# A three-part fused kernel on one core: the bonus term of the recurrence as two dense products with ones from unit 6 on, and a few moved steps

## The chip, the cores and the metric

The kernel runs on one core of a Trainium2 chip. The metric is the device time of one execution in microseconds (us), as the median of several runs. The engines are called PE (matrix products), DVE (vector), ACT (scalar), POOL (GpSimd) and SP (which here issues nearly all DMAs). Each runs its own list of instructions in order and waits on semaphores.

## The reference

Three blocks follow each other, all in float32, with batch B = 2, 8 heads, S = 768 steps, head size D = 48 (8 x 48 = 384 = DM), DFF = 1024.

```
for t in range(S):                       # recurrence, per batch and head
    y[t]  = r[t] @ (state + outer(u * k[t], v[t]))
    state = w[t][:, None] * state + outer(k[t], v[t])
x = y of all heads, side by side         # (B, S, 384)

xk, xr = mu * x + (1 - mu) * x_prev      # two mixes with the step before
out1   = sigmoid(xr @ w_r) * (relu(xk @ w_k) ** 2 @ w_v)

h = gelu(out1 @ w_in);  u2, v2 = halves of h
v2 = layernorm(v2) * g;  v2 = w_sg @ v2 + b_sg      # mixes the 768 steps
result = out1 + (u2 * v2) @ w_out
```

The part of y[t] that comes from u is, per head, (sum over d of r[t,d] * u[d] * k[t,d]) times v[t]: one number per step and head, times a vector. This is what the kernel calls the bonus.

## The kernel before

**Units.** The recurrence is cut into 12 units: unit `un` is a chunk of C = 128 steps (`un // 2`) of one batch (`un % 2`). The 8 heads lie as 4 pairs; a pair fills the 128 partitions, each head in a slot of 64 (48 used, the rest zero). One operand of a unit is thus 128 x 512: 4 pairs side by side, 128 steps each. For each unit DVE runs two scans over the decays (`scan`: prod, suffix) and makes k_in and r_in from them; PE makes the scores (`scores`), the keys by step (`keys_by_step`, a transpose), the bonus (`bonus`), the part of the state (`from_state`), the new state (`add_state`) and the part of the chunk (`from_chunk`). `outputs` is bonus, from_state, add_state, from_chunk. DVE masks the scores (`mask`), multiplies the bonus by v (`bonus`), adds the outputs (`last_output`, `main_output`) and carries the state on (`carry_on`). The outputs of a pair's last part go through small DMAs into X.

**The bonus before.** POOL multiplies r by k (`products`, L577) into rkp. PE multiplies rkp from the left by a matrix that repeats u along its columns (`u_b`, part of the tile par), so that every row of the result holds the sum: 8 products a unit, one for each pair and head, 64 x 64 weights and 64 x 128 moving columns, in plain float32 (L694). The result goes to bank pkt, for units 0, 1 and 3 to other banks.

**Split numbers.** The large products of the second and third block are made of three products of float32r numbers each: a number is split in a high part (rounded by ACT) and a low part (number minus high, by POOL or DVE), and high x high, high x low, low x high are added. The groups named `_h` and `_l` are these. `low_part` and `low_half` make the low parts of weights, `key_low` those of the squared activations k2.

**Stages.** The first feed-forward block goes in 6 stages s of 256 columns (chunk s of both batches). A stage has tiles RS (2), KS (4), VS (2) in `first_mlp`. While stage s runs on PE, the units a = 2s+2 and b = 2s+3 are made, and mix(s+1) (ACT and DVE) prepares the inputs of the next stage out of X. So units 6 and 7 belong to stage 2, 10 and 11 to stage 4, and the bonus of unit 6 comes right after RS[0] of stage 2. Stage 5 has no unit. After it the third block follows (L323 to L325 on PE).

**Order.** Everything is in an order written out by hand for each engine: a loop over the stages with one branch for s = 0, s = 1, the middle stages and the last. Each helper begins with its waits. What waits is the whole engine: an ACT instruction that waits for POOL holds back what stands behind it on ACT.

## Time and profile before

| | us |
|---|---|
| median of 3 runs | 326.71 (326.59 to 328.05) |
| the profiled execution, device time | 327.06 |
| its span, first to last instruction | 325.3 |
| PE busy | 317.0 (97%), 2682 instructions |
| DVE busy | 197.6 (61%), 340 instructions |
| ACT busy | 151.4 (47%), 304 instructions |
| POOL busy | 94.2 (29%), 92 instructions |

A row of the timeline gives start, length, engine, line, what is written and read, and in square brackets the idle time in front of it with what ended it; rows of the same kind are merged ("x16"). Matmuls overlap: the length of one is from its first step to its last result (268 ns for one of L694), while the next starts 64 ns later. What a run of them costs is therefore read from start to start, or from the chain of waits, which gives each group only the time up to the next one. A float32 product appears as two records. The device time is 1.8 us above the span.

### The profile page before, as it was taken

How to read it: one execution, taken by the hardware profiler on the slowest of the kernel's cores; microseconds unless marked ns; L12 is line 12 of the kernel's file. 1: busy time of each engine (PE TensorE's matmuls, PEld its weight loads, DVE VectorE, ACT ScalarE, POOL GpSimd, SP SyncE). 2: the span in 40 equal slices, each digit the busy share in tenths (PEclk: the TensorE clock that was granted, in tenths of full speed). 3: DMA queues.
4: the chain of work that ended last, by engine and by line, in shares of the span. 5: the costliest groups of instructions: out<-in, count | busy, mean ns of one | idle time of the engine just before them, and what ended most of it. 6: DMA issues, size and time to landing. Idle time of an engine off the chain costs nothing.

```text
span 325.3 us, 6820 instructions
## 1 busy us (share of the span) xinstructions
PE 317.0 (97%) x2682; PEld 298.7 (92%) x2682; DVE 197.6 (61%) x340; ACT 151.4 (47%) x304; POOL 94.2 (29%) x92
## 2 busy tenths in 40 slices
PE   6989999999999999999999999999999999999996
PEld 2769889998999999999999998899999989999995
DVE  5979997979985498549217156982535456123332
ACT  6478805742554655385555884744113026311100
POOL 5430140263014301431131141671333019213220
PEclk9999999999999999999999999999999999999999
DMA  7996044004413403200024055000000300000012
GB/s 230 406 390 264 3 169 170 2 13 166 163 33 138 168 3 93 88 0 2 8 78 174 0 200 190 2 0 0 2 0 3 121 24 0 2 0 2 0 48 97
DMA packets 11172, 28.07 MB, mean 86 GB/s; under 512 B 1216, under 2 KB 6016, under 8 KB 9856
## 3 DMA queue, kind: packets, MB, share of 16 engines
q1 hardware_dynamic: 10848, 27.33, 23.7%
q8 instruction: 21, 0.34, 0.4%
q10 hardware_dynamic: 288, 0.27, 0.3%
q14 instruction: 15, 0.12, 0.1%
HBM read 24.74 MB, written 2.36 MB: 83 GB/s over the span
## 4 chain that ended last, share of the span: by engine, by line
PE 93%; DVE 3%; ACT 1%; issue 1%; POOL 1%; DVEq 0%; ACTq 0%; POOLq 0%
PE dense L780 35%; PE dense L325 5%; PE dense L323 5%; PE dense L324 5%; PE ps L665 4%; PE ps L323 3%; PE ps L325 3%; PE ps L324 3%; PE pkt L694 3%; PE py L734 3%; PE py L748 3%; PE dense L319 2%; PE pu L718 2%; PE pkt L323 2%; PE pkt L325 2%; PE pu L323 2%
## 5 line engine op out<-in xcount | busy, mean ns | idle before, releaser
L586 POOL TENSOR_TENSOR k_l<-sq,k_h 128x512 fp32r<-128x512 f32 x22 | 28.3, 1292 | 58.0 <-ACT sq L1045 58.0
L577 POOL TENSOR_TENSOR rkp<-inw 128x512 f32<-128x512 f32 x12 | 16.2, 1352 | 81.9 <-DVE r_in L1275 61.6
L780 PE MATMUL dense<-k_h,wv_h 128*128 128x256 f32 x144 | 39.1, 286 | 0.0
L780 PE MATMUL dense<-xkr_h,wk_h 128*128 128x256 f32 x144 | 38.7, 291 | 0.0
L780 PE MATMUL dense<-k_h,wv_l 128*128 128x256 f32 x144 | 38.7, 283 | 0.0
L780 PE MATMUL dense<-xkr_h,wk_l 128*128 128x256 f32 x144 | 36.1, 283 | 0.0
L780 PE MATMUL dense<-k_l,wv_h 128*128 128x256 f32 x144 | 32.9, 283 | 0.0
L780 PE MATMUL dense<-xkr_l,wk_h 128*128 128x256 f32 x144 | 30.4, 283 | 0.0
L645 POOL TENSOR_TENSOR gated_l<-gf,gated_h 128x384 fp32r<-128x384 f32 x16 | 16.4, 1025 | 46.1 <-ACT gated_h L1174 36.2
L1174 ACT CAST gated_h<-gf 128x384 fp32r<-128x384 f32 x16 | 8.2, 513 | 42.9 <-DVE gf L1523 42.9
L780 PEld LDWEIGHTS dense<-xkr_h,wk_h 128*128 128x128 f32 x144 | 27.5, 191 | 0.6 <-issue 0.2
L780 PEld LDWEIGHTS dense<-k_h,wv_h 128*128 128x128 f32 x144 | 27.6, 192 | 0.3 <-issue 0.2
L780 PEld LDWEIGHTS dense<-k_h,wv_l 128*128 128x128 f32 x144 | 27.6, 192 | 0.0
L780 PEld LDWEIGHTS dense<-xkr_h,wk_l 128*128 128x128 f32 x144 | 26.7, 192 | 0.0
L1336 DVE SCALAR_TENSOR_TENSOR xf<-X,omu,xf 128x256 f32<-128x256 f32 x36 | 18.8, 536 | 12.6 <-ACT xf L1003 12.6
L1037 ACT ACTIVATE relu<-dense 128x512 f32<-128x512 f32 x24 | 14.3, 595 | 25.3 <-PE dense L780 25.3
L780 PEld LDWEIGHTS dense<-k_l,wv_h 128*128 128x128 f32 x144 | 24.2, 192 | 0.0
L1003 ACT ACTIVATE xf<-X,par 128x256 f32<-128x256 f32 x36 | 17.6, 504 | 13.0 <-DMA X<-y 11.3
L780 PEld LDWEIGHTS dense<-xkr_l,wk_h 128*128 128x128 f32 x144 | 23.3, 192 | 0.0
L619 POOL TENSOR_TENSOR rstd<-vare,half_neg 128x1 f32<-128x1 f32 x12 | 9.3, 777 | 29.8 <-DVE vare L1501 29.8
L627 POOL TENSOR_TENSOR vn_l<-vf,vn_h 128x512 fp32r<-128x512 f32 x12 | 17.1, 1430 | 2.2 <-ACT vn_h L1135 2.2
L1013 ACT CAST xkr_h<-xf 128x256 fp32r<-128x256 f32 x36 | 14.3, 397 | 6.4 <-DVE xf L1336 6.4
(258 smaller groups left out, 876.0 us busy)
## 6 DMA issues: line engine op xcount, KB each, us to landing
inw<-in_units SPq DMA_DIRECT2D x10, 1026.5 KB, 5.4
vb<-in_vT SPq DMA_DIRECT2D x12, 256.0 KB, 5.9
wsg_raw<-in_wsgT SPq DMA_DIRECT2D x1, 2304.0 KB, 8.8
out_y<-y_out SPq DMA_DIRECT2D x12, 192.0 KB, 1.9
wk_raw<-in_moe_w_k SPq DMA_DIRECT2D x3, 512.0 KB, 9.7
wv_raw<-in_moe_w_v SPq DMA_DIRECT2D x4, 384.0 KB, 15.1
win_raw<-in_moe_w_in SPq DMA_DIRECT2D x3, 512.0 KB, 4.7
inw<-in_units SPq DMA_DIRECT2D x2, 512.0 KB, 5.2
```

The source lines that it names most:

```text
L323: pe.matmul(o, a_h, b_h, start=first and n == 0, stop=False, skip_group_check=True)
L324: pe.matmul(o, a_h, b_l, start=False, stop=False, skip_group_check=True)
L325: mm = pe.matmul(o, a_l, b_h, start=False, stop=last and n == len(pairs) - 1, skip_group_check=True)
L577: pool.tensor_tensor(rkp[:, un % 2], inw[:, un % 3, W1:W1 + WIDE], inw[:, un % 3, W1 + WIDE:W1 + 2 * WIDE], ALU.mult).then_inc(rkp_done, 1)
L586: pool.tensor_tensor(k2_l[:, 2 * n:2 * n + 2], sq[:, j % 2].rearrange("p (g t) -> p g t", g=2), k2_h[:, 2 * n:2 * n + 2], ALU.subtract).th ...
L627: pool.tensor_tensor(vn_l[:, t], vf[:, n % 2], vn_h[:, t], ALU.subtract).then_inc(vnl_done, 1)
L645: pool.tensor_tensor(gated_l[:, x, cols], gf[:, ng % 2], gated_h[:, x, cols], ALU.subtract).then_inc(gl_done, 1)
L780: return pe.matmul(pm[bk][:, n * T:(n + 1) * T], weight[:, t, cols], inputs[:, t], start=first, stop=last, skip_group_check=True)
L1003: act.activation(batches(xf[:, kt, n]), X[:, s % 2, kt, :, 1:C + 1], ACT.Identity, scale=mu[:, n, kt:kt + 1]).then_inc(t_done, 1)
L1013: act.copy(xkr_h[:, n, kt], xf[:, kt, n]).then_inc(xh_done, 1)
L1037: act.activation(relu[:, j % 2], pm[bk][:], ACT.Relu).then_inc(m_free[bk], 1)
L1336: dve.scalar_tensor_tensor(out=batches(xf[:, kt, n]), in0=X[:, s % 2, kt, :, 0:C], scalar=omu[:, n, kt:kt + 1], in1=batches(xf[:, kt, n]), ...
```

## The change

Four things are changed.

- From unit 6 on (WIDE_FROM = 3 * N = 6) POOL multiplies r by u (read with a repeated column) and then by k; ACT rounds the result to rk_h, POOL takes the rest rk_l = rkp - rk_h, written over rkp; PE then multiplies rk_h and rk_l, 128 x 512 each, by `heads`, a 128 x 128 matrix with ones where row and column belong to the same head and zeros elsewhere. These are two float32r products that add up in bank pkt. ACT writes heads once, in stage 0.
- PE: the bonus of unit 1 stands in front of move_last(0), and the keys of unit 3 in front of its bonus.
- DVE: the low parts of wv and the two carries carry_on(0), carry_on(1) stand later; one half of the low part of wk goes from DVE to POOL; one wait of unit 0's scan is placed an instruction later.
- Room: rk_h lies over `moves`, which is used in units 0 and 1 alone; p_sum, of a branch that does not run here, lies over z.

The diff, without some lines of the layout and the declarations:

```diff
--- before
+++ after
@@ SBUF layout
+        rk_at = e
         rkp, e = put("rkp", e, [2, WIDE])
+        rk_l, _ = put("rk_l", rk_at, [2, WIDE], FR)
...
-        moves, e = put("moves", e, [KT, P])
+        moves, _ = put("moves", e, [KT, P])
+        rk_h, e = put("rk_h", e, [2, WIDE], FR)
+        heads, e = put("heads", e, [P], FR)
...
@@ which engine splits which weight tile
-        POOL_LOWS = [("wr", 0, 0), ("wk", 0, 0)]
-        DVE_LOWS = [("wk", 1, 0), ("wk", 2, 0), ("wk", 0, 1), ("wk", 1, 1), ("wk", 2, 1)]
+        POOL_LOWS = [("wr", 0, 0), ("wk", 0, 0), ("wk", 0, 1)]
+        DVE_LOWS = [("wk", 1, 0), ("wk", 2, 0), ("wk", 1, 1), ("wk", 2, 1)]
@@ POOL
+            def weighted(un):
+
+                n = un - WIDE_FROM
+                pool.wait_ge(s_par, 16)
+                pool.wait_ge(rin_done, un + 1)
+                pool.wait_ge(c_mm, un - 1)
+                pool.tensor_tensor(blocks(rkp[:, un % 2]), blocks(inw[:, un % 3, W1:W1 + WIDE]),
+                                   u_b[:, :, 0:1].to_broadcast([P, PAIRS, C]), ALU.mult).then_inc(rku_done, 1)
+                pool.wait_ge(rku_done, n + 1)
+                pool.tensor_tensor(rkp[:, un % 2], rkp[:, un % 2],
+                                   inw[:, un % 3, W1 + WIDE:W1 + 2 * WIDE], ALU.mult).then_inc(rkp_done, 1)
+
+            def weighted_low(un):
+                pool.wait_ge(rkh_done, un - WIDE_FROM + 1)
+                pool.tensor_tensor(rk_l[:, un % 2], rkp[:, un % 2], rk_h[:, un % 2], ALU.subtract).then_inc(rkl_done, 1)
...
-            low_half(pool, parts_of("wk")[0], 0, wl_done)
+            for half in range(2):
+                low_half(pool, parts_of("wk")[0], half, wl_done)
...
-            products(6)
+            weighted(6)
             key_low(1, KG - 1)
-            products(7)
+            weighted_low(6)
             for s in range(2, STAGES):
+                a, b = 2 * s + 2, 2 * s + 3
+                if b < NU:
+                    weighted(b)
+                    weighted_low(b)
                 key_low(s, 0)
-                if 2 * s + 4 < NU:
-                    products(2 * s + 4)
-                for n in range(1, KG):
+                if a + 2 < NU:
+                    weighted(a + 2)
+                key_low(s, 1)
+                if a + 2 < NU:
+                    weighted_low(a + 2)
+                for n in range(2, KG):
                     key_low(s, n)
-                if 2 * s + 5 < NU:
-                    products(2 * s + 5)
@@ PE, bonus
+                if un >= WIDE_FROM:
+                    pe.wait_ge(heads_done, 4)
+                    pe.wait_ge(rkh_done, un - WIDE_FROM + 1)
+                    pe.wait_ge(rkl_done, un - WIDE_FROM + 1)
+                    pe.matmul(pkt[:], heads[:], rk_h[:, un % 2], start=True, stop=False)
+                    pe.matmul(pkt[:], heads[:], rk_l[:, un % 2], start=False, stop=True).then_inc(c_mm, 1)
+                    return
@@ PE, order
             scores(1)
+            bonus(1)
             move_last(0)
-            bonus(1)
...
                     scores(b)
+                    keys_by_step(b)
                     bonus(b)
-                    keys_by_step(b)
@@ ACT
+            def all_heads():
+
+                for h in range(2):
+                    for i in range(2):
+                        at = slice(h * SLOT, (h + 1) * SLOT), slice(i * SLOT, (i + 1) * SLOT)
+                        act.activation(heads[at], ident[at], ACT.Identity, scale=0.0,
+                                       bias=ones[at[0], 0:1] if h == i else 0.0).then_inc(heads_done, 1)
+
+            def weighted_high(un):
+                act.wait_ge(rkp_done, un + 1)
+                act.wait_ge(c_mm, un - 1)
+                act.copy(rk_h[:, un % 2], rkp[:, un % 2]).then_inc(rkh_done, 1)
...
                     flag_out(s + 1)
+                    act.wait_ge(moved_mm, N)
+                    all_heads()
                     mix(s + 1)
...
                     flag_out(s + 1)
+                    weighted_high(b + 1)
                     mix(s + 1)
...
                     check(b)
+                    weighted_high(b)
                     gate(s, *RS[1])
                     keys(b)
                     key_high(s, 0)
                     flag_out(s + 1)
-                    for n in range(1, KG):
+                    key_high(s, 1)
+                    if a + 2 < NU:
+                        weighted_high(a + 2)
+                    for n in range(2, KG):
                         key_high(s, n)
@@ DVE
-                    dve.wait_ge(half_done, 1)
...
+                else:
+                    dve.wait_ge(half_done, 1)
...
             mask(1)
-            carry_on(0)
             bonus(1)
             last_output(1)
+            carry_on(0)
...
             mix(0)
-            carry_on(1)
-            for j in parts_of("wk"):
+            for j in parts_of("wk")[1:]:
                 low_half(dve, j, 1, wl2_done)
...
                     scan(a)
-                    low_part(dve, wv[0], wl2_done)
+                    carry_on(1)
                     key_low(0)
...
                     mask(b)
+                    low_part(dve, wv[0], wl2_done)
+                    bonus(b)
                     low_part(dve, wv[1], wl2_done)
-                    bonus(b)
-                    low_part(dve, wv[2], wl2_done)
                     output(b)
                     choose(s + 1)
+                    low_part(dve, wv[2], wl2_done)
                     low_part(dve, wv[3], wl2_done)
```

What stands on PE in stage 2 around the bonus of unit 6, before and then after; pkt is the bank, par holds u_b:

```order
L780 MATMUL dense<-xkr_l,wr_h 128x256
L694 MATMUL pkt<-rkp,par 64x128 [waits ktok_done,bonus_done,rkp_done,s_par]
L694 MATMUL pkt<-rkp,par 64x128 x7
L734 MATMUL py<-r_in,state 64x128 [waits main_done,y_done,state_done]
L734 MATMUL py<-r_in,state 64x128 x7
```

```order
L817 MATMUL dense<-xkr_l,wr_h 128x256
L724 MATMUL pkt<-rk_h,heads 128x512 [waits heads_done,bonus_done,rkh_done,ktok_done,rkl_done,rkp_done,s_par]
L725 MATMUL pkt<-rk_l,heads 128x512
L771 MATMUL py<-r_in,state 64x128 [waits main_done,y_done,state_done]
L771 MATMUL py<-r_in,state 64x128 x7
```

Eight products have become two, at the same place, with three more semaphores to wait for; the same stands there for the units 7 to 11.

POOL from the low part of key tile 2 of stage 1 to the end of stage 2, before and then after (k_l is key_low, rkp is products or weighted, rk_l is weighted_low):

```order
L577 TENSOR_TENSOR rkp<-inw 128x512 [waits c_mm,rin_done]
L586 TENSOR_TENSOR k_l<-sq,k_h 128x512 [waits k2h_done,sq_done]
L577 TENSOR_TENSOR rkp<-inw 128x512 [waits c_mm,rin_done]
L586 TENSOR_TENSOR k_l<-sq,k_h 128x512 [waits m_full0,k2h_done,sq_done]
L577 TENSOR_TENSOR rkp<-inw 128x512 [waits c_mm,rin_done]
L586 TENSOR_TENSOR k_l<-sq,k_h 128x512 [waits k2h_done,sq_done] x3
```

```order
L594 TENSOR_TENSOR rkp<-inw,par 128x512 [waits c_mm,rin_done,s_par]
L597 TENSOR_TENSOR rkp<-rkp,inw 128x512 [waits rku_done]
L610 TENSOR_TENSOR k_l<-sq,k_h 128x512 [waits k2h_done,sq_done]
L602 TENSOR_TENSOR rk_l<-rkp,rk_h 128x512 [waits rkh_done]
L594 TENSOR_TENSOR rkp<-inw,par 128x512 [waits c_mm,rin_done,s_par]
L597 TENSOR_TENSOR rkp<-rkp,inw 128x512 [waits rku_done]
L602 TENSOR_TENSOR rk_l<-rkp,rk_h 128x512 [waits rkh_done]
L610 TENSOR_TENSOR k_l<-sq,k_h 128x512 [waits m_full0,k2h_done,sq_done]
L594 TENSOR_TENSOR rkp<-inw,par 128x512 [waits c_mm,rin_done,s_par]
L597 TENSOR_TENSOR rkp<-rkp,inw 128x512 [waits rku_done]
L610 TENSOR_TENSOR k_l<-sq,k_h 128x512 [waits k2h_done,sq_done]
L602 TENSOR_TENSOR rk_l<-rkp,rk_h 128x512 [waits rkh_done]
```

Each unit has three POOL instructions instead of one, and the last of them waits for ACT.

DVE behind mix(0), around the scan of unit 2, before and then after:

```order
L371 TENSOR_TENSOR wk_l<-wk_raw,wk_h 128x512 [waits wh_done]
L1308 TENSOR_TENSOR state<-pu,prod 128x256 [waits u_mm]
L371 TENSOR_TENSOR wk_l<-wk_raw,wk_h 128x512 [waits wh_done] x3
L1241 SCALAR_TENSOR_TENSOR prod<-inw,one 128x516 [waits state_done,s_in2]
L1254 RECIPROCAL ends<-prod 128x4 [waits suffix_done,prod_done]
L1262 SCALAR_TENSOR_TENSOR suffix<-inw,ends 128x516 [waits kin_done,inv_done]
L1270 TENSOR_TENSOR k_in<-inw,suffix 128x512 [waits kt_mm,sc_mm,suffix_done]
L1275 TENSOR_TENSOR r_in<-inw,prod 128x512 [waits y_mm]
L364 TENSOR_TENSOR wv_l<-wv_raw,wv_h 128x768 [waits wh_done]
L1367 TENSOR_TENSOR k_l<-sq,k_h 128x512 [waits k2h_done,sq_done]
```

```order
L379 TENSOR_TENSOR wk_l<-wk_raw,wk_h 128x512 [waits wh_done] x3
L1298 SCALAR_TENSOR_TENSOR prod<-inw,one 128x516 [waits state_done,s_in2]
L1312 RECIPROCAL ends<-prod 128x4 [waits suffix_done,prod_done]
L1320 SCALAR_TENSOR_TENSOR suffix<-inw,ends 128x516 [waits kin_done,inv_done]
L1328 TENSOR_TENSOR k_in<-inw,suffix 128x512 [waits kt_mm,sc_mm,suffix_done]
L1333 TENSOR_TENSOR r_in<-inw,prod 128x512 [waits y_mm]
L1366 TENSOR_TENSOR state<-pu,prod 128x256 [waits u_mm]
L1425 TENSOR_TENSOR k_l<-sq,k_h 128x512 [waits k2h_done,sq_done]
```

One low part and the carry of unit 1 no longer stand in front of the scan of unit 2, and the first low part of wv no longer stands behind it.

## Rows read from the trace of the kernel before

**Rows 1.** The page: busy time of PE, and the chain that ended last by engine.

```profile
PE 317.0 (97%) x2682; PEld 298.7 (92%) x2682; DVE 197.6 (61%) x340; ACT 151.4 (47%) x304; POOL 94.2 (29%) x92
...
PE 93%; DVE 3%; ACT 1%; issue 1%; POOL 1%; DVEq 0%; ACTq 0%; POOLq 0%
```

**Rows 2.** The waits of PE: who waited for whom, us, times, longest.

```profile
PE dense L319 <- POOL upper L566: 2.9, 1, 2.9
...
PE dense L780 <- ACT xkr_h L1013: 1.1, 1, 1.1
...
PE ps L665 <- DVE k_in L1270: 1.0, 1, 1.0
```

**Rows 3.** Chain of waits, bonus of unit 6: start us, us, what.

```profile
89.86 1.02 PE pkt L694 x16
```

**Rows 4.** All records of L694 from 80 to 170 us; the last is unit 11's.

```profile
L694 PE MATMUL pkt<-rkp,par x96: 268/270/321, 89.8 to 162.1; 64*64 64x128 f32 x96
```

**Rows 5.** Timeline of PE, float32r products of 512 columns.

```profile
197.74 0.39 PE L323 MATMUL ps<-win_h,x_h 128*128 128x512 f32 x1
...
199.83 0.39 PE L323 MATMUL ps<-win_h,x_h 128*128 128x512 f32 x1
```

**Rows 6.** Chain of waits, plain float32 product of 512 columns (two records).

```profile
10.36 1.05 PE dense L319 x2
```

**Rows 7.** Timeline of POOL, stage 2.

```profile
90.53 1.28 POOL L577 TENSOR_TENSOR rkp<-inw 128x512 f32<-128x512 f32 x1 [11.31 <-DVE r_in L1275]
...
101.30 1.28 POOL L577 TENSOR_TENSOR rkp<-inw 128x512 f32<-128x512 f32 x1
...
109.36 1.29 POOL L586 TENSOR_TENSOR k_l<-sq,k_h 128x512 fp32r<-128x512 f32 x1 [5.54 <-ACT sq L1045]
```

**Rows 8.** Timeline of ACT, stage 2: end of the checks, second gate, a cast of 128x512.

```profile
93.42 0.19 ACT L980 ACTIVATION_READ_ACCUMULATOR junk<-junk,minus_one 128x1 f32 x1
95.63 0.38 ACT L1027 ACTIVATE x<-dense 128x256 f32<-128x256 f32 x1 [2.03 <-PE dense L780]
...
98.84 0.63 ACT L1041 ACTIVATE k_h<-relu 128x512 fp32r<-128x512 f32 x1
```

**Rows 9.** Chain of waits, bonus of unit 7, and VS[1] with RS[0] of stage 3.

```profile
100.65 1.02 PE pkt L694 x16
...
115.82 5.03 PE dense L780 x42
```

**Rows 10.** Timelines of POOL and ACT at the end of stage 1.

```profile
76.70 1.27 POOL L577 TENSOR_TENSOR rkp<-inw 128x512 f32<-128x512 f32 x1 [5.62 <-DVE r_in L1275]
...
80.92 0.91 ACT L1003 ACTIVATE xf<-X,par 128x256 f32<-128x256 f32 x2 [5.38 <-DMA X<-y]
```

**Rows 11.** Timeline of ACT, mix(3): first input of the gates of stage 3.

```profile
113.13 0.41 ACT L1013 CAST xkr_h<-xf 128x256 fp32r<-128x256 f32 x1 [0.89 <-DVE xf L1336]
```

**Rows 12.** Timelines of DVE and POOL: a DVE line beside POOL work.

```profile
42.06 1.15 DVE L1308 TENSOR_TENSOR state<-z,prod 128x256 f32<-128x256 f32 x1
...
41.67 2.68 POOL L586 TENSOR_TENSOR k_l<-sq,k_h 128x512 fp32r<-128x512 f32 x2
```

**Rows 13.** Timeline of DVE in front of the scan of unit 2.

```profile
26.85 0.42 DVE L1308 TENSOR_TENSOR state<-pu,prod 128x256 f32<-128x256 f32 x1
27.18 1.89 DVE L371 TENSOR_TENSOR wk_l<-wk_raw,wk_h 128x512 fp32r<-128x512 f32 x3
```

**Rows 14.** Timeline of PE: move_last(1), scores of unit 2, bonus of unit 3.

```profile
18.09 0.91 PE L759 MATMUL py<-y,moves 128*128 128x128 f32 x6 [0.16 <-DVE y L1317]
...
33.12 1.16 PE L665 MATMUL ps<-r_in,k_in 64*128 64x128 f32 x16 [0.96 <-DVE k_in L1270]
...
41.81 1.09 PE L694 MATMUL dense<-rkp,par 64*64 64x128 f32 x16 [0.24 <-issue]
```

**Rows 15.** Timeline of DVE, mask of unit 3 and the low part behind it.

```profile
43.14 1.34 DVE L1282 COPY_PREDICATED att<-upper,ps 128x1024 f32<-128x1024 uint32 x1
44.38 0.94 DVE L364 TENSOR_TENSOR wv_l<-wv_raw,wv_h 128x768 fp32r<-128x768 f32 x1
```

More of the change, by code:

```diff
@@ L90, in build @@
         state, e = put("state", e, [2, PAIRS, SLOT])
+        z_at = e
         z, e = put("z", e, [PAIRS, SLOT])
         y3, e = put("y3", e, [2, C])
-        moves, e = put("moves", e, [KT, P])
+        moves, _ = put("moves", e, [KT, P])
+        rk_h, e = put("rk_h", e, [2, WIDE], FR)
+        heads, e = put("heads", e, [P], FR)
         junk, e = put("junk", e, [PAIRS, C])
@@ L148, in build @@
         p_kv, e = put("p_kv", e, [PAIRS, D])
-        p_sum, e = put("p_sum", e, [PAIRS, D])
+        p_sum, _ = put("p_sum", z_at, [PAIRS, D])
         p_u, e = put("p_u", e, [PAIRS, D])
@@ L223, in build @@
             "prod_done", "inv_done", "suffix_done", "rkp_done", "rin_done", "kin_done"))
+        rku_done, rkh_done, rkl_done, heads_done = (sem(n) for n in ("rku_done", "rkh_done", "rkl_done", "heads_done"))
         c_mm, kt_mm, sc_mm, u_mm, y_mm, flag_mm, last_mm, moved_mm = (sem(n) for n in (
@@ L289, in build @@
         HANDED = 2
+        WIDE_FROM = 3 * N
         def given(eng, s):
```

## The prediction

> **What bounds the kernel now.** I read the page first. PE is busy for 317.0 of 325.3 us, and the chain of work that ended last lies on PE for 93% [rows 1]. The view of the waits then shows what PE waits for: 2.9 us at the start, 1.1 us for the first input of the gates, 1.0 us for k_in [rows 2]. The first is untouched. So the kernel is bound by what PE has to do, step after step: an edit on PE counts in full, an edit on DVE, ACT or POOL counts only where PE waits for it, or where it makes PE wait. The granted clock of TensorE is 0.999 over the span, its level of 2.4 GHz, so no stretch is slow for that reason.
>
> Third, the chain of waits gives the price of one bonus on PE: 1.02 us from its start to the start of from_state, for 16 records of 64 ns [rows 3]. The records of L694 between 80 and 170 us are 96, six units of 16 [rows 4]: these are the units 6 to 11.
>
> **The wide bonus on PE.** Removed are six times 1.02 us, 6.1 us. Added are six pairs of float32r products with 512 moving columns. The kernel has such products in its third block, and nine of them go from 197.74 to 199.83, 0.232 us each from start to start [rows 5]. A pair is 0.46 us, and the difference 0.56 us a unit, 3.3 us for six. Those nine are loaded with new weights each time, and the load is hidden there; here both use the same heads. From the other side, the nearest plain float32 row of this width is 1.05 us for one product [rows 6]; if heads and rk went at that rate, a pair would be 2.1 us and the change would lose 1.08 us a unit, 6.5 us. I take 0.46: form, width and number type agree with [rows 5] in all points. For the change from one kind of product to the next I allow nothing, since at this place the bonus starts now without a gap behind RS[0].
>
> **Does the wide bonus come in time?** It needs rk_l, the end of a chain that is longer: POOL twice 1.28, ACT a cast of about 0.63, POOL 1.29, about 4.5 us with the gaps, where 1.28 us did before. What PE waits for is this chain against the place of the bonus.
> - Units 7, 9, 11: r_in is ready at 90.5 in stage 2, where POOL's only instruction starts [rows 7]. Both products end at 93.1. ACT has its checks until 93.6 [rows 8] and does the cast to 94.2, before the second gate at 95.6; POOL ends rk_l at 95.6. PE wants it at 100.65 [rows 9]: 5 us to spare. Behind the waiting cast on ACT stand gate(RS[1]) and keys(7); neither is late.
> - Units 8, 10: POOL starts at 101.3 [rows 7], ends both at 103.9, then the low part of key tile 1, then rk_l until about 106.5. The bonus of unit 8 is behind RS[0] of the next stage, near 120.9; POOL's next own work is at 109.4 [rows 7], behind a wait for ACT. Nothing is held back. key_low(1) ends 1.3 us later, at 105.2; its reader, VS[0] of the stage, is behind the last two key tiles.
> - Unit 6: POOL starts at 76.7 and ends both products at 79.3; ACT casts to 79.9 in front of mix(2), whose first row waits for a DMA until 80.92 [rows 10]. 1.0 us to spare, and mix itself is not urgent (below). key_low(3) of stage 1 ends at 80.5; VS[0] started at 78.45 and wants it at its seventh of eight steps, at 82.7.
> - heads: four ACT instructions of 64 x 64 in stage 0, in front of mix(1). I put them at 0.2 to 0.4 us each, between the one-column and the 256-column instructions of ACT, together 0.8 to 1.6; ACT idles there for the DMA into X, as it does in stage 1 for 5.38 us [rows 10]. Nothing.
>
> **Twelve more POOL instructions beside DVE.** A state line of DVE took 1.15 us where POOL worked on k_l [rows 12], and 0.42 us at the same line without [rows 13]: it lay still until POOL's instruction was over. DVE can thus lose up to 1.3 us for each added POOL instruction. The chain that matters is output, DMA, mix, RS[0] of the next stage. For stage 3 the first xkr_h is ready at 113.5 [rows 11]; VS[1] and RS[0] are 42 products from 115.82 over 5.03 us, and the last 18 of them begin at 118.7 [rows 9]. That is 5.2 us to spare, and one lock of 1.3 us, or two, are inside. DVE's scans stand behind mix with 2.8 us to spare (r_in at 90.5 [rows 7]; the scores of unit 7 start at 93.2, by the chain 3.4 us behind the start of the bonus of unit 6 [rows 3]). I cost the locks at 0 and keep 0.6 us for the range.
>
> The Trainium skill speaks against the change just here: SBUF — State Buffer, section Who interferes with whom, says that a DVE instruction with two SBUF inputs and a GpSimd instruction that reads SBUF shut each other out for the whole instruction. By that rule the state lines, scans and mixes are held up by every added POOL instruction they meet, bonus, mask and outputs (one operand in PSUM) by none. The trace agrees: the 1.15 us row has both operands in SBUF.
>
> **The front.** On DVE one low part of wk and carry_on(1) leave the place before the scan of unit 2: 0.33 us for the carry (26.85 to 27.18) and a third of 1.8 us for the low part, 0.6 [rows 13], together 0.93. PE idles 0.96 us there, for k_in [rows 14]. Its own work is over at 32.0, so about 0.9 comes back. POOL gets the low part at 18.7 to 20.0, where it idles until 34.4. What is late next: the scores of unit 3. They start at 39.4 by the new count, and r_in of unit 3 is ready at about 39.3 (the low part of wv no longer stands in front, the carry of 0.4 does). Just in time. Behind them the bonus of unit 3 waits 0.24 us for POOL [rows 14]; with the keys in front that is covered, 0.2 back. The scan of unit 0 loses a wait, but PE is still in its first products then: 0. bonus(1) before move_last(0) lets DVE read it in time, and move_last(1), which waits 0.16 [rows 14], starts with it about 0.1 earlier; PE waits for X there, so 0.1. Sum 1.2. Its ends: 0 if new waits eat it, 1.4 if all three rows vanish.
>
> The low parts of wv are the cover that gets thin. The mask of unit 3 would end at 43.5, a low part takes 0.94 [rows 15], and VS[0] starts at 44.9 and wants a further one every 1.44 us (12 products of 0.12). They are ready at 44.4, 45.9, 47.5 and 48.4 for 44.9, 46.3, 47.7 and 49.2: 0.2 to 0.8 us to spare. If output(3) is late by 0.5, PE waits 0.3.
>
> **Sum.** 3.3 + 1.2 = 4.5 us off the profiled execution: its span goes to 320.8, its device time from 327.06 to 322.6. The median of the runs is 0.35 lower than that execution, and 326.71 - 4.5 = 322.2. I forecast **322.3**. The third block is PE's throughout and only moves forward.
>
> **Rivals.**
> - *The front gives nothing.* scan(3), or the low parts of wv, come late and take the 0.9 to 1.2 us back; for it speaks that r_in and scores meet within 0.1 us. 326.7 - 3.3 = 323.4.
> - *The locks or the long chain bite.* POOL and DVE hold each other up more than the rows say, or each pair has a gap of 0.2 to 0.3 us before or behind it on PE. Six times 0.3 is 1.8, so 324.1. Against it: the spare times of 2.8 to 5.2 us, and [rows 5] without gaps.
> - *The pair does not pay at all.* The products with heads are done in a way that costs like eight narrow ones; only the front is left, 325.5.
> - *Slower.* The place is the pair on PE, the mechanism its rate: at the 1.05 us of [rows 6] for each product it costs 2.1 instead of 1.02, and 326.7 + 6.5 - 1.2 = 332.0. It decides from 0.61 us a product on, where six pairs cost 1.2 us more than before and eat the front. Against it stand all float32r rows of the third block.
>
> **Chances.** Forecast 0.66 (its own range 321.4 to 323.0), front 0.16, locks and gaps 0.10, no gain from the pair 0.04, slower 0.04. A measurement of this kernel tells about 0.5% from no change, 1.6 us: the first three cases are faster, 0.91 with a part of the third near the bound; no change 0.05, slower 0.04. The range that holds 8 of 10 takes in the first two and part of the third: 321.2 to 324.2.
>
> **What would show it.** Right: two records of 128x512 per unit from heads, 0.46 us to the start of from_state; PE's wait for k_in at unit 2 gone; no new PE wait in stages 2 to 4; rk_l written 4 us and more before its product. Wrong: a pair of over 0.6 us; PE waiting for POOL rk_l or ACT rk_h; RS[0] waiting for xkr_h; VS[0] of stage 0 waiting for wv_l.

## The result

The changed kernel takes 324.31 us (median of 7 runs, 323.13 to 325.0) against 327.09 us before (7 runs on the same chip, 326.59 to 328.05). The ratio is 0.991, with an interval of 0.9895 to 0.9926: 2.4 to 3.4 us less, where 4.5 were forecast. The time lies 0.1 us above the upper end of the forecast range (324.2). The range was set from a median of 326.71 us for the kernel before (3 runs), and that median is 327.09 here; the ratio taken of 326.71 gives 323.8, inside the range. The gain is what came out too small: 2.8 us. The profiled execution took 324.56 us, with a span of 322.8 us.

### The profile page after: what moved, and what is told of

Its sections match the earlier page's. It is cut to its first block, busy times and chain, and to the rows that moved or that the text cites. A ratio compares the mean times of both kernels' runs of the same rounds, so it can differ in the third digit from the quotient of the medians.

```text
span 322.8 us, 6686 instructions
## 1 busy us (share of the span) xinstructions
PE 314.5 (97%) x2598; PEld 294.8 (91%) x2598; DVE 199.3 (62%) x339; ACT 155.6 (48%) x314; POOL 109.4 (34%) x105
## 4 chain that ended last, share of the span: by engine, by line
PE 90%; DVE 5%; issue 1%; DMA 1%; ACT 1%; POOL 1%; SPq 0%; DVEq 0%; ACTq 0%; POOLq 0%
PE dense L817 35%; PE dense L332 5%; PE dense L331 5%; PE dense L333 5%; PE ps L695 3%; PE ps L332 3%; PE ps L331 3%; PE ps L333 3%; PE py L771 2%; PE py L785 2%; PE dense L327 2%; PE pkt L331 2%; PE pkt L332 2%; PE pkt L333 2%; PE pu L332 2%; PE pu L331 2%
## 5 line engine op out<-in xcount | busy, mean ns | idle before, releaser
L585 POOL TENSOR_TENSOR rkp<-inw 128x512 f32<-128x512 f32 x6 | 8.6, 1426 | 46.7 <-DVE r_in L1333 29.0
```

## The profile after

The page, busy time and the chain by engine, as in [rows 1]:

```profile
PE 314.5 (97%) x2598; PEld 294.8 (91%) x2598; DVE 199.3 (62%) x339; ACT 155.6 (48%) x314; POOL 109.4 (34%) x105
...
PE 90%; DVE 5%; issue 1%; DMA 1%; ACT 1%; POOL 1%; SPq 0%; DVEq 0%; ACTq 0%; POOLq 0%
```

PE has 84 records fewer: 96 narrow ones went and 12 wide ones came. The chain leaves PE more often than before (90% against 93%), although PE was to wait less. So a new wait has to be looked for. The waits of PE, as in [rows 2] (who waited for whom, us in total, times, longest):

```profile
PE dense L327 <- POOL upper L574: 2.9, 1, 2.9
PE dense L817 <- ACT xkr_h L1063: 1.1, 1, 1.1
PE ps L695 <- issue: 0.5, 2, 0.3
PE dense L817 <- DVE x L1433: 0.5, 1, 0.5
PE pu L740 <- DVE state L1366: 0.2, 1, 0.2
PE py L796 <- PE py L785: 0.2, 1, 0.2
```

The wait for k_in is gone, as forecast. Three others have come: 0.5 us in two pieces before scores, 0.5 us for DVE in the feed-forward block, and 0.2 us for the state at the flag's product. The last row is the old wait of move_last(1), 0.16 us in both kernels, with another releaser. In time:

```profile
31.76 1.16 PE L695 MATMUL ps<-r_in,k_in 64*128 64x128 f32 x16
...
38.98 1.16 PE L695 MATMUL ps<-r_in,k_in 64*128 64x128 f32 x16
...
41.92 0.19 PE L740 MATMUL pu<-outside,ones 128*1 128x4 f32 x2 [0.17 <-DVE state L1366]
...
57.22 0.38 PE L817 MATMUL dense<-xkr_h,wk_h 128*128 128x256 f32 x1 [0.45 <-DVE x L1433]
...
62.02 1.16 PE L695 MATMUL ps<-r_in,k_in 64*128 64x128 f32 x16 [0.23 <-issue]
...
77.18 1.16 PE L695 MATMUL ps<-r_in,k_in 64*128 64x128 f32 x16 [0.28 <-issue]
```

The first two rows are the scores of units 2 and 3; neither waits, so "just in time" held. The row at 41.92 is the flag's product. The last three rows lie in stages 1 and 2, where no new wait was forecast. The chain of waits shows where they come from: the second small copy into X of unit 3 (start us, us, what).

```profile
46.02 0.57 SPq L460
46.59 0.05 issue
46.64 3.87 DMA X<-y
```

mix(1) on ACT waits for that copy. From the issue of the pair of copies at 46.02 to the first row of mix at 50.67 it takes 4.65 us here. In the profile of before it is 47.47 to 50.16, 2.69 us. So the copies are issued 1.45 us earlier than before, and mix starts 0.5 us later.

The wide bonus of unit 6 in the chain of waits, as in [rows 3]:

```profile
89.75 0.23 PE pkt L724
89.98 0.23 PE pkt L725
90.21 1.02 PE py L771 x16
```

The pair costs 0.46 us, exactly as read from [rows 5]. But from_state (L771) behind it takes 1.02 us. Grouped by line from 80 to 170 us, first in the kernel after, then in the kernel before (busy us, mean ns of one):

```profile
L771 PE MATMUL py<-r_in,state 64*64 64x128 f32 x96 | 6.5, 275 | 0.0
```

```profile
L694 PE MATMUL pkt<-rkp,par 64*64 64x128 f32 x96 | 6.5, 276 | 0.0
L734 PE MATMUL py<-r_in,state 64*64 64x128 f32 x96 | 6.2, 269 | 0.0
```

Before, the bonus (L694) had the higher mean and from_state (L734) the lower one. Now from_state has the higher one. POOL's chain for units 6 and 7, as in [rows 7, 10]:

```profile
77.21 1.04 POOL L594 TENSOR_TENSOR rkp<-inw,par 128x512 f32<-128x512 f32 x1 [5.60 <-issue]
78.33 1.09 POOL L597 TENSOR_TENSOR rkp<-rkp,inw 128x512 f32<-128x512 f32 x1
...
80.82 1.29 POOL L602 TENSOR_TENSOR rk_l<-rkp,rk_h 128x512 fp32r<-128x512 f32 x1
91.22 1.05 POOL L594 TENSOR_TENSOR rkp<-inw,par 128x512 f32<-128x512 f32 x1 [9.11 <-issue]
92.35 1.09 POOL L597 TENSOR_TENSOR rkp<-rkp,inw 128x512 f32<-128x512 f32 x1
94.17 1.37 POOL L602 TENSOR_TENSOR rk_l<-rkp,rk_h 128x512 fp32r<-128x512 f32 x1 [0.73 <-ACT rk_h L1040]
```

rk_l of unit 7 is done at 95.5 (forecast 95.6), and the pair of products that reads it starts at 100.0; rk_l of unit 6 is done at 82.1, and its pair starts at 89.75 in the chain above. No PE row waits for rk_h, rk_l or heads. The four ACT instructions for heads lie at 42.3 to 43.3 us, in the idle time in front of mix(1).

One more thing has to be taken out before traces are compared: the start-up. In front of the first scores PE runs four products whose result is not used (`warm(pe, 4)`, eight records). They need a different time in each execution: the scores of unit 0 start at 8.49 us in the profile of before, at 7.97 in this one, and up to 9.56 in others. The Trainium skill says the same of a kernel's first products (TensorE: Matmul & The Clock Gate, section What's actually happening): how many of them go at the slow rate varies from run to run. The traces agree: the same eight records take 5.16 to 6.75 us. In the nine profiles with four such products the first four records start 0.85 to 1.02 us apart, the later ones from some record on 0.43; in three of the nine all eight are slow. So I compare from the start of scores(0) to the end of the span. Before: 8.49 to 325.3, 316.8 us. After: 7.97 to 322.8, 314.8 us.

## The experiments

Twelve runs were made, in three sets of four: after_again, wide_only, front_only and x_before_load; state_first, after_look, x_look and three_warm; the last four. Those of a set ran on one chip beside runs of the kernel before, whose medians were 327.09, 327.82 and 327.5 us. "Net" is the time from the start of scores(0) to the end of the span in the profile of that kernel. "Copy to mix" is the time from the issue of the two copies into X of unit 3 to the first row of mix(1).

| kernel | median us (range, runs) | ratio to before (interval) | scores(0) starts | net | copy to mix |
|---|---|---|---|---|---|
| before | 327.09 (326.59 to 328.05, 7) | | 8.49 | 316.8 | 2.69 |
| after | 324.31 (323.13 to 325.0, 7) | 0.991 (0.9895 to 0.9926) | 7.97 | 314.8 | 4.65 |
| after_again | 325.24 (323.38 to 325.91, 6) | 0.9938 (0.9916 to 0.996) | 8.23 | 313.5 | 2.75 |
| wide_only | 325.07 (324.23 to 325.73, 6) | 0.9931 (0.9912 to 0.995) | 9.54 | 314.5 | 2.75 |
| front_only | 326.39 (325.58 to 327.05, 12) | 0.9972 (0.9959 to 0.9985) | 8.07 | 316.8 | 4.23 |
| x_before_load | 324.59 (323.73 to 325.0, 6) | 0.9916 (0.9898 to 0.9935) | 9.42 | 313.5 | 2.77 |
| state_first | 328.0 (1) | | 9.45 | 316.9 | 2.69 |
| after_look | 324.67 (1) | | 9.54 | 313.5 | 2.74 |
| x_look | 324.67 (1) | | 9.56 | 313.4 | 2.75 |
| three_warm | 323.05 (322.87 to 323.79, 5) | 0.9867 (0.9846 to 0.9888) | 7.74 | 313.5 | 2.75 |
| two_warm | 324.45 (322.97 to 324.92, 6) | 0.9897 (0.9878 to 0.9917) | 7.82 | 315.4 | 2.73 |
| three_no_wait | 323.81 (322.87 to 324.34, 5) | 0.9893 (0.9877 to 0.9909) | 7.72 | 313.5 | 2.75 |
| three_no_wait_look | 322.92 (1) | | 7.74 | 313.5 | 2.76 |
| three_warm_look | 323.04 (1) | | 7.88 | 313.4 | 2.75 |

The net column comes from one profiled execution for each row; it is far steadier than the medians. It is 316.8 to 316.9 for the two kernels without either half of the change (before, state_first), and 313.4 to 313.5 for the eight profiles with both halves, four products or three in front, and mix(1) starting in time. The changed kernel itself has the medians 324.31 in its first set and 325.24 in the next, which is 2.8 and 1.85 us under the kernel before.

### after_again: the changed kernel once more

No edit.

> The changed kernel, once more. In its profile the last small transfer of unit 3 into X landed 3.9 us after its issue, where the others took 2.0. Theory chance: here it lands after 2.0, mix(1) starts near 48.8 instead of 50.7, PE does not wait for DVE x at 57.2, and the span is about 1 us shorter than 322.8. Theory fixed: it lands late again, at about the same place, and the span is 322.8 within 0.5. Median under both 323.5 to 324.5.

Measured: 325.24 us, and in the profile copy to mix is 2.75 us. The first row of mix(1), in this kernel and then in the profile of the kernel after:

```profile
49.01 0.91 ACT L1053 ACTIVATE xf<-X,par 128x256 f32<-128x256 f32 x2 [5.46 <-DMA X<-y]
```

```profile
50.67 0.91 ACT L1053 ACTIVATE xf<-X,par 128x256 f32<-128x256 f32 x2 [7.37 <-DMA X<-y]
```

The new waits of PE in stages 1 and 2 are gone in it, and net it is 313.5 us. So the late copy belongs to single executions, and it is worth 314.8 - 313.5 = 1.3 us (1.45 by scores(6) in the table below). Rows of waits account for 0.45 + 0.23 + 0.28 = 0.96 us of that.

Where each half gains can be read from the scores of later units. Counted from the start of scores(0), in us:

| | scores(2) | scores(4) | scores(6) |
|---|---|---|---|
| before | 24.63 | 53.98 | 68.79 |
| wide_only | | 53.97 | 68.79 |
| front_only (copy late) | 23.76 | 53.60 | 68.79 |
| after (copy late) | 23.79 | 54.05 | 69.21 |
| after_again | 23.77 | 52.95 | 67.76 |

scores(6) stands in front of the first wide bonus, so its column holds the front alone: 1.03 us gained with the copy in time.

### wide_only: the wide bonus without the moves of the front

The changed kernel, with the order of PE, DVE and POOL before unit 6 set back:

```
-            bonus(1)
-            move_last(0)
+            move_last(0)
+            bonus(1)
...
-                    keys_by_step(b)
-                    bonus(b)
+                    bonus(b)
+                    keys_by_step(b)
...
-            for j in parts_of("wk")[1:]:
+            carry_on(1)
+            for j in parts_of("wk"):
```

> The kernel before with the wide bonus alone; all moves of the first 50 us undone. Theory of the switch (the first group of narrow products behind dense ones pays 0.15 us; the bonus paid it, now from_state does): 6 x 0.41 = 2.5 us less than before, 324.5 against 327.0; from_state 1.02 instead of 0.87 us in the units 6 to 11. By the prediction's 0.56 a unit: 3.3 us less, 323.7.

Measured: 325.07 us, and net 314.5, 2.3 us under the kernel before. The chain at unit 6:

```profile
90.92 0.23 PE pkt L723
91.15 0.23 PE pkt L724
91.38 1.02 PE py L770 x16
```

The row of from_state (L770) has the 1.02 us here too, so it does not come from the moves. A unit saves 1.02 + 0.87 - 0.46 - 1.02 = 0.41 us, six units 2.5 us, against 2.3 net.

### front_only: the moves without the wide bonus

The kernel before with the edits of wide_only the other way round.

> The kernel before with the moves of the first 50 us alone, bonus as before. If the late transfer into X is the reason that they gain nothing: with a late landing again 0 to 0.3 us less than before (326.8), with a landing after 2.0 us 1.0 to 1.2 less (325.9). Rival, DVE's chain gives it back anyway (scan of unit 4 against the scores of unit 4): 0 to 0.3 less with a landing after 2.0 us too.

Measured: 326.39 us, ratio 0.9972 with an interval of 0.9959 to 0.9985: 0.4 to 1.3 us faster. The profile shows no net gain, 316.8 us. But copy to mix was 4.23 us in it, and the two waits at the scores that came with the late copy in after are there; the one for DVE in the feed-forward block is not. The 0.2 us at the flag's product belongs to the front itself, since after_again has it too. The 1.1 us is the old wait for the first input of the gates. From the waits of PE in it:

```profile
PE dense L781 <- ACT xkr_h L1014: 1.1, 1, 1.1
PE ps L666 <- issue: 0.5, 2, 0.3
PE pu L704 <- DVE state L1310: 0.2, 1, 0.2
```

By the table above it was 0.87 us ahead of the kernel before at scores(2) and level with it at scores(6), so that execution gives back what the front gained. The gain itself reads from the two halves: 314.5 (wide_only) minus 313.5 (both, copy in time) is 1.0 us, as scores(6) has it. The medians of this set do not show it on top of the wide bonus: 325.07 (wide_only) and 325.24 (after_again), with intervals that overlap.

### x_before_load, x_look: the copies into X before the next load

In after, SP issues the load of unit 6 (1 MB) at 48.19 us, while the copy is still under way. The edit makes SP wait for the copies first:

```
                     if un + 2 >= 4 and un + 2 < NU:
+                        if s and un == 2 * s + 2:
+                            sp.wait_ge(x_in, 16 * HANDED * N * s)
                         load_unit(un + 2)
```

> The changed kernel, and SP waits for all transfers into X before it issues the load of the first unit of the next stage (units 6, 8, 10). Theory that this load of 1 MB holds the last small transfer up: it lands after 2.0 us in stage 0, PE's waits for DVE x and at the scores of unit 4 go, 0.7 to 1.1 us less than the changed kernel. Theory that the load has nothing to do with it: no difference within 0.3 us, and the landing as before.

Measured: 324.59 us, net 313.5, copy to mix 2.77 us. The copy was in time, but the median does not differ clearly from that of the changed kernel: it is 325.24 in the same set (after_again) and 324.31 in the first, and the intervals of the ratios cover each other. Two more profiles, one of each kernel:

> The changed kernel, with SP waiting for the copies into X before it issues the load of unit 6, one more profile. Theory 1 (the load behind it slows the copy): the copy lands 1.9 to 2.1 us after issue, as it did the first time, and PE waits for nothing at stage 1. Theory 2 (chance, whatever is behind it): a landing of 3.5 us or more is as likely here as in the changed kernel.

> The changed kernel itself, one more profile. It is taken for one row: how long the second copy into X of unit 3 lies between issue (about 46.6 us) and landing. Theory 1 (with the front moved forward the copy meets the load of unit 6 that follows it on the queue, each time): 3.5 to 3.9 us, and PE waits 0.4 to 0.5 us at first_mlp of stage 1. Theory 2 (chance, one of several executions): as likely 1.9 to 2.1 us with no wait of PE behind it.

Measured: in time in both, 2.75 and 2.74 us. With after_again this makes one late copy in three profiles of after. The claim that the load behind the copy slows it each time has fallen; that it does so in some executions is not excluded.

### state_first: who pays the 0.15 us

The kernel before, with the narrow bonus of units 6 to 11 behind from_state:

```
-                bonus(un)
+                if un < 6:
+                    bonus(un)
...
                 from_state(un)
+                if un >= 6:
+                    bonus(un)
```

> The kernel before, with the eight narrow bonus products of units 6 to 11 moved behind from_state, so that from_state stands right behind the dense products of RS[0]. Theory 1 (the first group of narrow fp32 products behind dense ones pays 0.15 us, whichever group it is): from_state takes 1.02 us where it took 0.87, the bonus 0.87 to 0.88 where it took 1.02, the pair of them 1.89 as before; the device time stays at that of the kernel before. Theory 2 (the bonus is dearer by itself, and the 1.02 of from_state behind the wide pair is what heads, rk_h or rk_l do to it): the bonus stays at 1.02 and from_state at 0.87. Theory 3 (the 0.15 hangs on the change of the tile's shape between bonus and state products): both at 1.02, the pair at 2.04.

Measured: 328.0 us (one run), net 316.9. The chain at unit 6:

```profile
90.83 1.02 PE py L734 x16
91.85 0.87 PE pkt L694 x16
```

By line, 80 to 170 us:

```profile
L734 PE MATMUL py<-r_in,state 64*64 64x128 f32 x96 | 6.5, 275 | 0.0
L694 PE MATMUL pkt<-rkp,par 64*64 64x128 f32 x96 | 6.2, 269 | 0.0
```

The two lines have exchanged their times, and the pair is 1.89 us as before. So neither product is dearer by itself. The first group of 16 narrow float32 products behind dense ones takes 1.02 us, the next 0.87. Theory 1 stands and the others fall.

The dense products are not the only ones that bring it. The chain of waits of the kernel before, at units 5 and 6:

```profile
73.58 1.02 PE pkt L694 x16
74.60 0.12 PE pu L703 x2
74.72 1.02 PE py L734 x16
...
89.86 1.02 PE pkt L694 x16
90.88 0.87 PE py L734 x16
```

At unit 5 the flag's product (L703) stands between the two groups, one product with 128x1 weights in plain float32, and from_state pays the 0.15 us too. So a change between float32r and plain float32 is not needed for it. What the cases have in common is that the product in front has weights of another shape than 64x64; that this is the cause is likely, and what PE does in the 0.15 us is not shown.

### three_warm, three_warm_look: a shorter start-up

In the profiles with four unused products, scores(0) starts between 7.97 and 9.56 us, while r_in of unit 0 is ready at 7.5 to 7.7 in those with the front moved. x_before_load with one product less:

```
-            warm(pe, 4)
+            warm(pe, 3)
```

> The changed kernel with the wait of SP before the load of unit 6, and with three instead of four products in front of scores(0) (they only keep TensorE at work; their result is not used). In the profiles so far the eight records of these four products end at 7.97 to 9.42 us, and r_in of unit 0 is ready at 7.55 to 7.69. Theory 1 (PE's start is bound by those products, since the front lost a wait on DVE): six records end by 7.6 to 8.5, scores(0) starts at 7.7 to 8.5, and the device time falls by 0.3 to 0.9 us against the same kernel with four (324.59), to 323.7 to 324.3. Theory 2 (the fourth product is what brings TensorE to its fast records): the records of scores(0) come at a slower rate, and the time is the same or up to 1 us longer.

Measured: 323.05 us, ratio 0.9867 (0.9846 to 0.9888). This interval lies below those of after and of x_before_load, so the kernel is faster than both, and its median is the lowest of the timed kernels. The timeline of PE, first of after_look with four products, then of three_warm:

```profile
2.88 6.74 PE L327 MATMUL dense<-one,ident 128*128 128x512 f32 x8 [2.88 <-POOL upper L574]
9.54 1.16 PE L695 MATMUL ps<-r_in,k_in 64*128 64x128 f32 x16
```

```profile
2.88 4.58 PE L327 MATMUL dense<-one,ident 128*128 128x512 f32 x6 [2.88 <-POOL upper L576]
7.74 1.16 PE L697 MATMUL ps<-r_in,k_in 64*128 64x128 f32 x16 [0.28 <-DVE r_in L1335]
```

The scores now wait for r_in, not for the unused products. The net time is 313.5 as with four, so the whole gain is the start-up. One thing stays open: in all four profiles with three products the records reach the fast spacing by 7.3 us, but in five of the nine with four products not before 8.9. What three products do in such an execution no profile shows. A second profile gave 323.04 us and 7.88:

> three_warm (with the wait of SP) once more, one profile, for the same row: 1.9 to 2.1 us by both theories if the wait of SP is what helps; 3.5 us or more in this one would show that a copy lands late with no load behind it.

### two_warm: one product less again

```
-            warm(pe, 3)
+            warm(pe, 2)
```

> three_warm with two products in front of scores(0). In three_warm scores(0) waits 0.28 us for r_in of unit 0 at 7.74 us. Theory 1 (those products only have to last until r_in; TensorE's rate has settled by then): four records end at 5.5 to 6.5, PE idles about 1.3 to 2.2 us for r_in, scores(0) starts at 7.7 as in three_warm, and the time stays at 323.0, within 0.3. Theory 2 (an idle PE before scores(0) brings slow records back): scores(0) and what follows it go at half the rate for a while, and the time is 1 to 3 us above three_warm, 324 to 326.

Measured: 324.45 us (322.97 to 324.92). The slow scores of theory 2 are there in the profiled execution; its reason is not shown, as follows below. The lowest run is as fast as those of three_warm, so two products seem to do in some executions. The timeline of PE:

```profile
2.87 3.78 PE L327 MATMUL dense<-one,ident 128*128 128x512 f32 x4 [2.87 <-POOL upper L576]
7.82 2.08 PE L697 MATMUL ps<-r_in,k_in 64*128 64x128 f32 x16 [1.16 <-DVE r_in L1335]
9.83 1.11 PE L708 MATMUL pkt<-ident,k_in 128*128 128x128 f32 x4
```

PE idles 1.16 us before the scores. Their 16 records then take 2.08 us instead of 1.16, and the four transposes 1.11 instead of 0.66. But the four records in front of the idle time start at 2.87, 3.89, 4.74 and 5.60, all at the slow spacing. They had not become fast before PE idled, so this profile does not show that idle time brings slow records back: the slow scores may simply continue what was slow before. Net it is 315.4, 1.9 us more than with three. The granted clock stands at 1.00 in every one of these stretches, its level of 2.4 GHz. So these slow records do not show in that column, only in the durations and in the spacing.

### three_no_wait, three_no_wait_look: three products without the wait of SP

x_before_load's edit taken out of three_warm again.

> The changed kernel with three products in front of scores(0) and without the wait of SP before the load of unit 6. So far the second copy into X of unit 3 landed late (3.5 and 3.9 us) in two of four profiles with the front moved and no such wait, both of executions with a short start-up, and in none of three with the wait. Theory 1 (a short start-up puts the copy where the load behind it reaches it): late, 3.5 us or more, PE waits 0.4 us or more at stage 1, and the median is 0.3 to 1.3 us above three_warm (323.05). Theory 2 (chance of one execution, the wait does nothing): 2.0 us, and the median is that of three_warm within 0.3.

> three_no_wait once more, one profile. Theory 1: the copy lands 3.5 us or more after issue here too. Theory 2: 1.9 to 2.1 us in one of the two at least.

Measured: copy to mix is 2.75 and 2.76 us, in time in both. The median of 323.81 lies 0.8 above that of three_warm, but its lowest run is 322.87 as there, and the intervals of the ratios overlap a little (0.9877 to 0.9909 against 0.9846 to 0.9888). In all, the copy was late in two of six profiles with the front moved and no wait of SP, and in none of five with the wait (x_before_load, x_look, three_warm, three_warm_look, two_warm). Theory 1 of this pair, late at each short start-up, has fallen. Whether the wait of SP prevents a late copy or not, these counts can't tell. One more row goes with it: SP issues the two copies of the unit before (unit 2) in 1.32 us in both late profiles, and in 1.80 to 2.06 us in the nine with the front moved and the copy in time. In the three profiles without the moved front it is 1.32 too, with the copy in time. This is a lead and not a cause.

## Why the forecast was right in direction and too large

**The pair on PE: right.** 0.23 + 0.23 us from start to start, no plain float32 rate. The rival "slower" and the rival "does not pay" fall with it.

**"For the change from one kind of product to the next I allow nothing": wrong.** This is the step that failed, and the largest part of the miss. The reason given was that the bonus already started without a gap behind RS[0]. There was no gap, but the price was inside the bonus: its 1.02 us held 0.15 us that whichever narrow group comes first behind the dense products pays, which state_first shows. When the bonus goes, the next narrow group inherits it. Removed were thus 0.87 us a unit, not 1.02, and the term is 0.41 x 6 = 2.5 us instead of 3.3. It could have been read: from_state, with the same shape and count, took 0.87 us right behind the bonus in the profile of before, against the bonus's 1.02, and 1.02 where the flag's product stood between them.

**The front: right in mechanism, 1.0 instead of 1.2 us.** The wait of 0.96 for k_in and the 0.24 in front of bonus 3 are gone, and scores(3) do not wait. New is 0.17 us at the flag's product: it follows the bonus directly now, and DVE's state line ends that much later. 0.96 + 0.24 - 0.17 = 1.03, and scores(6) of after_again come 1.03 us earlier than before. The 0.1 us put down for move_last(1) did not come: it still waits 0.16 us. The low parts of wv come in time, thin cover or not.

**The long chain over POOL and ACT: right.** rk_l within 0.1 us of the forecast for unit 7, nobody waits for it. The first POOL instruction, with u broadcast, took 1.04 to 1.05 us rather than the 1.28 I had put down, and the second 1.09 to 1.28.

**The locks: hardly more than before, and without a price.** DVE's rows around 80 us, first in the kernel before, then in the kernel after:

```profile
78.58 0.92 DVE L1308 TENSOR_TENSOR state<-z,prod 128x256 f32<-128x256 f32 x1
80.96 0.17 DVE L1350 COPY X<-X 128x6 f32<-128x6 f32 x1 [0.18 <-DMA X<-y]
```

```profile
78.83 0.87 DVE L1366 TENSOR_TENSOR state<-z,prod 128x256 f32<-128x256 f32 x1
81.28 0.87 DVE L1408 COPY X<-X 128x6 f32<-128x6 f32 x1 [0.28 <-DMA X<-y]
```

The state line takes 0.42 us alone. It was held up here in both kernels for about the same time: before, it lies beside POOL's k_l (77.93 to 79.21), after, beside the added product of POOL (L597, 78.33 to 79.42). Another row of it, 1.36 us at 70.54 in the kernel after, lies beside POOL's k_l, which also stands in both; front_only, which has none of the added POOL instructions, has it with 1.38. Only the small copy is slower than in the kernel before; it meets the added rk_l. The rule of the Trainium skill that I cited (SBUF — State Buffer, section Who interferes with whom) agrees for the state rows, with both operands in SBUF; the copy has one input, and the part of the rule that I cited does not cover it. No wait of PE follows from any of them. The spare times of 2.8 to 5.2 us are a sufficient reason, but no run took them away.

**What the forecast did not have: one execution is not like the next.** Its working took all from one profile of before, in which scores(0) started at 8.49 us and the copy was in time. With four unused products scores(0) started anywhere from 7.97 to 9.56 us, which alone moves the time by 1.6 us. The forecast read the granted clock of 0.999 as a sign that no stretch is slow; at the start records go at half their later rate while that column shows 1.00. The late copy adds 1.3 us where it happens. On equal terms (net) the change is worth 316.8 - 313.5 = 3.3 us: 4.5 minus 0.9 for the switch, minus 0.2 at the front, to within 0.1. The medians show 2.8 in the first set and 1.85 in the next. The 0.5 to 1.4 us between are probably what start-up and late copies do in the runs; only profiled runs show them, so this is not shown.

The range's end of 324.2 came from the case "locks and gaps", in which each pair has a gap of 0.2 to 0.3 us. Its size was nearly right (0.15 us), its form was not: no gap, and no lock, but a dearer neighbour. From the median that the range was set on, the result is inside it (323.8).

## What to carry to other kernels

When a group of products is removed, price it at what its like costs in the middle of a run of such products, not at what it costs in its own place: the surcharge of the first of its kind stays and moves to the next group. Before comparing two traces, cut off the start-up and look for one-off late transfers; a net time from the first real product on agreed to 0.1 us in eight profiles while the medians differed by over 2 us. And when an input comes earlier, look again at filler work in front of it: one unused product less took 1.5 us off the median from x_before_load to three_warm, and 0.5 to 1.4 us from the changed kernel (its two sets) to three_no_wait.

## What the runs showed of the hardware

- 16 products of 64x64 weights and 128 moving columns in float32 take 1.02 us as the first such group behind dense 128x128 products (state_first, after) or behind a single one with 128x1 weights (before), and 0.87 us behind another group of 64x64 (before, state_first), without an idle row between.
- A plain float32 product of 512 columns is two records. In all 14 profiles the first four records start 0.85 to 1.02 us apart, later ones 0.43. The change came between 6 and 9 us into the span, or, in three profiles with four products, not before they ended: their eight records took 5.16 to 6.75 us. In two_warm, with four records in front and 1.16 us of idle time behind them, the scores were slow as well. The granted clock was shown at 1.00 (2.4 GHz) throughout.
- Of two like copies into X of 24 KB, the second let mix start 2.69 to 2.77 us after the first one's issue in 12 of 14 profiles, but 4.65 us in one profile of after (it landed after 3.87 us) and 4.23 us in front_only. In after the DMA share was down to 0.04 from 48.5 to 49.0 us, so the DMA engines were not full for at least that part of the time that it was pending. The cause is open.
